# ScalarE writes the feature-128 term of every odd slice into PSUM; TensorE adds three products to it instead of making four

## What is computed

```
X = fft(fft(x, axis=1), axis=2).real          # (2, 3008, 256), seen as 6016 tokens
h = X @ w_in;  g = where(h > 0, h, exp(min(h, 0)) - 1);   y = g @ w_out        # 256 -> 2048 -> 256
h2 = y @ w2_in; g2 = max(h2, 0) + alpha * min(h2, 0);     out = g2 @ w2_out    # 256 -> 2048 -> 256
```

## Time and profile before

| | |
|---|---|
| median of 3 runs | 978.06 us (978.02 to 979.47) |
| the profiled execution | 977.41 us |
| its span in the trace | 975.6 us |
| TensorE busy (its matmuls) | 957.6 us, 98% of the span |
| VectorE busy | 793.1 us, 81% |
| ScalarE busy | 625.1 us, 64% |
| GpSimd busy | 169.9 us, 17% |
| first block, from its first up1 to the second block | 47.41 to 476.15 us |

### The profile page before, as it was taken

One profiled execution on the slowest core, in us unless ns is written; L12 is line 12 of the kernel. 1 busy time (PEld: TensorE's weight loads), 2 busy tenths in 40 slices (PEclk: granted clock), 3 DMA queues, 4 the chain that ended last, 5 costly groups with the idle time before them and its releaser, 6 DMA issues.

```text
span 975.6 us, 12207 instructions
## 1 busy us (share of the span) xinstructions
PE 957.6 (98%) x4450; PEld 798.1 (82%) x4450; DVE 793.1 (81%) x891; ACT 625.1 (64%) x816; POOL 169.9 (17%) x184
## 2 busy tenths in 40 slices
PE   7989999999999999999999999999999999999997
PEld 7868888888888888887888888888888888888886
DVE  6489897887887997889798888878879878887765
ACT  3378887887887787777665555555555555555453
POOL 3478231322321551027000000000000000000000
PEclk9999999999999999999999999999999999999999
DMA  9511120210212346231310110011011011000101
GB/s 245 148 42 36 63 79 1 98 43 29 70 44 98 130 151 243 92 119 44 108 38 1 44 43 1 1 44 44 1 44 43 1 39 44 1 1 1 43 1 44
DMA packets 11704, 57.57 MB, mean 59 GB/s; under 512 B 1706, under 2 KB 2666, under 8 KB 8060
## 3 DMA queue, kind: packets, MB, share of 16 engines
q1 hardware_dynamic: 7628, 30.80, 9.4%
q0 software_dynamic: 4016, 25.99, 7.3%
HBM read 32.75 MB, written 24.01 MB: 58 GB/s over the span
## 4 chain that ended last, share of the span: by engine, by line
PE 58%; DVE 2%; issue 1%; ACT 0%; DVEq 0%; ACTq 0%
PE ACC L604 9%; PE ACC L605 9%; PE ACC L606 9%; PE PQ L556 8%; PE PQ L557 8%; PE PQ L558 8%; PE ACC L574 2%; PE ACC L575 2%; PE ACC L579 2%; DVE Gl L884 1%; DVE G L861 1%; PE PQ L537 0%; PE PQ L538 0%; PE PQ L539 0%; PE PQ L543 0%
## 5 line engine op out<-in xcount | busy, mean ns | idle before, releaser
L574 PE MATMUL ACC<-Gh,W 128*128 128x512 f32 x372 | 144.9, 389 | 2.4 <-DVE Gl L884 2.3
L884 DVE SCALAR_TENSOR_TENSOR Gl<-G,Gh 128x1024 fp32r<-128x1024 f32 (+1 forms) x96 | 122.5, 1276 | 27.1 <-ACT Gh L709 26.3
L575 PE MATMUL ACC<-Gl,W 128*128 128x512 f32 x372 | 143.7, 386 | 0.0
L886 DVE TENSOR_TENSOR Gl<-G,Gh 128x1024 fp32r<-128x1024 f32 (+1 forms) x96 | 115.2, 1200 | 17.7 <-ACT Gh L711 17.3
L604 PE MATMUL ACC<-Gh,W 128*128 128x512 f32 x324 | 124.8, 385 | 2.1 <-DVE Gl L886 2.1
L861 DVE SCALAR_TENSOR_TENSOR G<-H,G 128x1024 f32<-128x1024 f32 (+1 forms) x96 | 125.8, 1311 | 1.0 <-ACT G L730 1.0
L711 ACT ACTIVATE Gh<-G 128x1024 fp32r<-128x1024 f32 (+1 forms) x96 | 100.3, 1045 | 39.9 <-DVE G L876 34.7
L606 PE MATMUL ACC<-Gh,W 128*128 128x512 f32 x324 | 124.5, 384 | 0.0
L605 PE MATMUL ACC<-Gl,W 128*128 128x512 f32 x324 | 124.5, 384 | 0.0
L876 DVE SCALAR_TENSOR_TENSOR G<-H,G 128x1024 f32<-128x1024 f32 (+1 forms) x96 | 115.5, 1204 | 3.3
L579 PE MATMUL ACC<-Gh,W 128*128 128x512 f32 x372 | 113.4, 386 | 0.0
(11 more groups left out here) (112 smaller groups left out, 1801.8 us busy)
## 6 DMA issues: line engine op xcount, KB each, us to landing
w_scratch<-stage POOLq DMA_DIRECT2D x4, 1792.0 KB, 7.2
xr<-in_x SPq DMA_DIRECT2D x16, 384.0 KB, 12.5
raw<-in_w POOLq DMA_DIRECT2D x24, 256.0 KB, 4.4
W3a<-w_scratch POOLq DMA_DIRECT2D x3, 1792.0 KB, 11.0
y_scratch<-y_st SPq DMA_DIRECT2D x5, 1024.0 KB, 3.9
y_in<-y_scratch SPq DMA_DIRECT2D x5, 1024.0 KB, 4.8
out_y<-y_st SPq DMA_DIRECT2D x5, 1024.0 KB, 3.9
w_scratch<-stage POOLq DMA_DIRECT2D x4, 1024.0 KB, 4.9
```

The lines of the kernel that those rows point to most:

```text
L574: mm(o, W2[:, f, 0, sl], Gh[:, j, c:c + w], start=f == 0, stop=False)
L575: mm(o, W2[:, f, 0, sl], Gl[:, j, c:c + w], start=False, stop=False)
L884: stt(Gl[:, j, 0:n], G[:, j, 0:n], bias, f32(Gh[:, j, 0:n]), ALU.add, ALU.subtract).then_inc(lo_ready, 1)
```

## The change

For odd f, ScalarE writes `eb * we` into `PQ[:, 1, 0:512]` before up1 (function `extra`): `eb` is the data row of feature 128 copied to all 128 partitions, `we` one weight per partition, both in full fp32. TensorE's three products then add to it with `start=False`, and L544 is left out. Even f keeps the fourth product. `W1e` holds half the slices. What is new at the start: a third row set (`e_row`) through DRAM and a broadcast load of it in each tile, the weights through DRAM into a column per slice (`load_we`), and a small add on GpSimd. The matmuls of the transforms get other `start` flags, with the same count and sizes.

```
+            def load_we(n, a, b):
+                odd = slice(a // 2, b // 2)
+                sp.wait_ge(w1l_ready, b)
+                sp.dma_start(we_dram[odd, :, :], f32(W1[0:1, a + 1:b:2, 2:4, :])).then_inc(we_stored[n], 16)
+                sp.wait_ge(we_stored[n], 16)
+                sp.dma_start(we_parts[:, odd, :], we_dram[odd, :, :].rearrange("f k p -> p f k"),
+                             allow_slow_non_contiguous=True).then_inc(we_in[n], 16)
+
+            load_we(0, 0, LATE_F)
             load_e(0)
             load_e(1)
+            load_we(1, LATE_F, NF)
...
                 gp.wait_ge(w1e_in, 48 * (n + 1))
+                gp.wait_ge(we_stored[n], 16)
                 gp.memset(f32(W1[0:1, a:b, 2:4, :]), 0.0).then_inc(w1_ready, 1)
+                gp.wait_ge(we_in[n], 16)
+                odd = slice(a // 2, b // 2)
+                gp.tensor_tensor(we[:, odd], we_parts[:, odd, 0], we_parts[:, odd, 1], ALU.add).then_inc(we_ready, 1)
...
-                mm(o, W1[:, f, 0, :], eo(t, 0), start=True, stop=False)
-                mm(o, W1[:, f, 0, :], eo(t, 2), start=False, stop=False)
-                mm(o, W1[:, f, 1, :], eo(t, 0), start=False, stop=False)
-                mm(o, W1e[:, f * PT:(f + 1) * PT], eo(t, 4), start=False, stop=True).then_inc(up_done, 1)
+                if j:
+                    pe.wait_ge(extra_ready, s // 2 + 1)
+                mm(o, W1[:, f, 0, :], eo(t, 0), start=not j, stop=False, skip_group_check=True)
+                mm(o, W1[:, f, 0, :], eo(t, 2), start=False, stop=False, skip_group_check=True)
+                ins = mm(o, W1[:, f, 1, :], eo(t, 0), start=False, stop=j == 1, skip_group_check=True)
+                if not j:
+                    ins = mm(o, W1e[:, f // 2, :], eo(t, 4), start=False, stop=True, skip_group_check=True)
+                ins.then_inc(up_done, 1)
...
+            def extra(s):
+                t, f = s // NF, s % NF
+                if f == 1:
+                    act.wait_ge(eb_in[t % 2], 16 * (t // 2 + 1))
+                if s == 1:
+                    act.wait_ge(we_ready, 1)
+                    act.wait_ge(eol_ready, 1)
+                if s > LATE_F and s - 2 < LATE_F:
+                    act.wait_ge(we_ready, 2)
+                if t < LAST and f == FLIP_AT[t]:
+                    act.wait_ge(eol_ready, t + 2)
+                if s >= 2:
+                    act.wait_ge(comb_ready, s - 1)
+                fn(PQ[:, 1, 0:TW], eb[:, t % 2, :], ACT.Copy, scale=we[:, f // 2:f // 2 + 1]).then_inc(extra_ready, 1)
...
+            extra(1)
             for s in range(S1):
...
                 neg(s)
+                if s % 2 and s + 2 < S1 and not flip_after:
+                    extra(s + 2)
```

More of the change, by code:

```diff
@@ L54, in program @@
     ALU, ACT = mybir.AluOpType, mybir.ActivationFunctionType
-    e_dram = nc.dram_tensor("e_scratch", [2, B * K2, N1], fp32).ap()
+    e_dram = nc.dram_tensor("e_scratch", [3, B * K2, N1], fp32).ap()
+    we_dram = nc.dram_tensor("we_scratch", [NF // 2, 2, PT], fp32).ap()
     y_dram = nc.dram_tensor("y_scratch", [NT, PT, YW], fp32).ap()
@@ L76, in program @@
     W1 = at("W1", o1, [PT, NF, 4, PT], f32r)
-    W1e = at("W1e", o1 + 32 * KB, [PT, F], f32r)
+    W1e = at("W1e", o1 + 32 * KB, [PT, NF // 2, PT], f32r)
+    eb = at("eb", o1 + 36 * KB, [PT, 2, TW], fp32)
     o2 = o1 + 40 * KB
@@ L125, in program @@
     warm = at("warm", o6 + 2048, [PT, 1], fp32)
+    we_parts = at("we_parts", o6 + 2304, [PT, NF // 2, 2], fp32)
+    we = at("we", o6 + 2368, [PT, NF // 2], fp32)
+    e_row = at("e_row", o6 + 2560, [C47 // 2, 2, N1], fp32)
     m64 = [mcf[:, cs * PT:(cs + 1) * PT] for cs in range(2)]
@@ L145, in program @@
         w1e_in, w1_ready, w2_ready = sem("w1e_in"), sem("w1_ready"), sem("w2_ready")
+        we_stored, we_in = [[sem(f"{name}{n}") for n in range(2)] for name in ("we_stored", "we_in")]
+        we_ready, eb_in, extra_ready = sem("we_ready"), [sem("eb_in0"), sem("eb_in1")], sem("extra_ready")
         raw_free, w3_stored, w4_stored, stage_ready = sem("raw_free"), sem("w3_stored"), sem("w4_stored"), sem("stage_ready")
@@ L150, in program @@
         f1_done, t1a_ready, t1b_ready = sem("f1_done"), sem("t1a_ready"), sem("t1b_ready")
-        u_done, uh_ready, ul_ready = sem("u_done"), sem("uh_ready"), sem("ul_ready")
+        u_done, uh_ready, ul_ready, uf_ready = sem("u_done"), sem("uh_ready"), sem("ul_ready"), sem("uf_ready")
         e_zero, e_stored, e_in = sem("e_zero"), sem("e_stored"), [sem("e_in0"), sem("e_in1")]
@@ L249, in _ @@
                 sp.dma_start(e_dram[part, two:two + B, :], f32(e_hl[0:B, part, 1, :])).then_inc(e_stored, 16)
-            sp.wait_ge(e_stored, 64)
+            sp.wait_ge(uf_ready, 2)
+            sp.dma_start(e_dram[2, 0:two, :], e_row[0:two, 0, :]).then_inc(e_stored, 16)
+            sp.dma_start(e_dram[2, two:two + B, :], e_row[0:B, 1, :]).then_inc(e_stored, 16)
+            sp.wait_ge(e_stored, 96)
             sp.wait_ge(e_zero, 1)
@@ L256, in load_e @@
                     sp.dma_start(f32(eo(t, 4)[p:p + 1, :]), src).then_inc(e_in[t % 2], 16)
+                src = e_dram[2, NQ * t:NQ * (t + 1), :].rearrange("q k -> (q k)").partition_broadcast(PT)
+                sp.dma_start(eb[:, t % 2, :], src).then_inc(eb_in[t % 2], 16)
+            def load_we(n, a, b):
[6 more added lines that the diff above has]
+            load_we(0, 0, LATE_F)
             load_e(0)
             load_e(1)
+            load_we(1, LATE_F, NF)
             for t in range(NT - 1):
@@ L322, in _ @@
             ins.then_inc(e_zero, 1)
-            chain(gp.memset(f32(W1e[:, :]), 0.0))
+            chain(gp.memset(f32(W1e[:, :, :]), 0.0))
             for c in range(4):
@@ L340, in move_row @@
                 for p, part in ((0, 2), (32, 3), (64, 2)):
-                    row = f32(W1e[p:p + 1, :]).rearrange("p (f c) -> p f c", f=NF)[:, a:b, :]
-                    gp.dma_start(row, f32(W1[0:1, a:b, part, :])).then_inc(w1e_in, 16)
+                    gp.dma_start(f32(W1e[p:p + 1, a // 2:b // 2, :]), f32(W1[0:1, a:b:2, part, :])).then_inc(w1e_in, 16)
                 gp.wait_ge(w1e_in, 48 * (n + 1))
+                gp.wait_ge(we_stored[n], 16)
                 gp.memset(f32(W1[0:1, a:b, 2:4, :]), 0.0).then_inc(w1_ready, 1)
+                gp.wait_ge(we_in[n], 16)
+                odd = slice(a // 2, b // 2)
+                gp.tensor_tensor(we[:, odd], we_parts[:, odd, 0], we_parts[:, odd, 1], ALU.add).then_inc(we_ready, 1)
             gp.wait_ge(w1l_ready, 2 * (FOLDS - LATE_FOLDS))
@@ L468, in flip1 @@
                         o = PQ[:, c % 2, k * PT:(k + 1) * PT]
-                        ins = mm(o, xr[:, c % XS, k * PT:(k + 1) * PT], m47[:, :], start=True, stop=True)
+                        ins = mm(o, xr[:, c % XS, k * PT:(k + 1) * PT], m47[:, :], start=k % XH == 0, stop=True,
+                                 skip_group_check=True)
                     ins.then_inc(f1_done, 1)
@@ L516, in flip2 @@
                     for n, (c, cs) in enumerate(parts):
-                        ins = mm(o, T1[:, c, :], m64[cs], start=n == 0, stop=n == len(parts) - 1)
+                        ins = mm(o, T1[:, c, :], m64[cs], start=q % (NQ // 2) == 0 and n == 0, stop=n == len(parts) - 1,
+                                 skip_group_check=True)
                 ins.then_inc(f2_done, 1)
@@ L689, in _ @@
                         fn(e_hl[0:r, 0, n, :], ACC[0:r, 0, o:o + N1], ACT.Copy).then_inc(uh_ready, 1)
+                        fn(e_row[0:r, n, :], ACC[0:r, 0, o:o + N1], ACT.Copy).then_inc(uf_ready, 1)
                 t1_copy(c)
@@ L738, in _ @@
                 flip_next = t < LAST and f == FLIP_AT[t] - 1
+                flip_after = t < LAST and f == FLIP_AT[t] - 2
                 if f == 2 and t:
@@ L751, in _ @@
                 if flip_next:
+                    if s % 2 == 0:
+                        extra(s + 1)
                     copy_q(s + 1)
@@ L834, in _ @@
                     dve.wait_ge(uh_ready, 2)
+                    dve.wait_ge(uf_ready, 2)
                     for n, (r, o) in enumerate(U_PARTS):
```

## The result

The changed kernel took 980.90 us (median of 11 runs, 979.37 to 981.80), the kernel before 978.54 beside it (11 runs, 977.17 to 981.10): ratio 1.0023, 95% interval 1.0014 to 1.0032. It is slower by about 2.4 us, where 976.6 was predicted and 0.09 given to "slower". The profiled execution took 981.02 us with a span of 979.2; that of before took 977.41 and 975.6.

What follows compares the result with a forecast made beforehand. TensorE was taken as the bound mid-block, VectorE as the bound or close to it at 60 to 80 and 440 to 460 us. 10.9 - 4.0 - 2.6 - 2.0 - 0.9 = 1.4 us, so 978.06 becomes 976.6; range 973.8 to 979.2.

Steps and rivals of the forecast that it cites:

- The saving of 0.226 a product: Odd slices of the first block: 48 removed TensorE products give back 0.226 us each, 10.9 us if TensorE is the bound.
- The instruction of 0.56: ScalarE's queue: each of 48 added 512-column activations takes 0.56 us, close to the nearest row, a copy from SBUF.
- The joints: Five hand-overs between tiles and four flips at f = 8, where slack is gone: 4.0 and 2.6 us lost.
- 0.79 each: Loss at each of five hand-overs between tiles: 0.56 of delay plus 0.23 of lost saving, 4.0 us in all.
- 0.66 each: Loss at each of four flips at f = 8: up1 0.35 later, 0.23 saving lost, 0.08 after a wait; 2.6 in all.
- The last tile: TensorE waits for g_lo: three odd slices give nothing (0.7), plus 0.2 for a later g_hi; 0.9 us lost.
- Tile 0: Start of the first block, VectorE the bound up to slice 8: 2.0 us of losses together.
- the 0.56 at down1(2): Tile 0, slice 2: g_hi stands behind the extra activation for slice 5, so down1 loses 0.56 us.
- The loads at nothing: Start: the new loads and broadcast cost nothing, with 11 us of cover before the first up1.
- No price for a wait inside a slice: TensorE's new semaphore before the fourth product costs zero; the rival had 0.08 us broken overlap, 979.0 us, chance 0.10.
- the joints absorb it: Rival: hand-overs and flips are not pushed or TensorE makes it up; 8.0 us gained, 970.1 us, chance 0.12.
- The second block as long as before: Profile after: the second block, whose code is the same, keeps its length.

Runs made afterwards that it cites:

- k1: Changed kernel with the extra activation moved at nine joints: behind eo_hi and copy_q at flips, behind exp_neg at hand-overs; 976.38 us, ratio 0.9978.
- k11: Changed kernel with the extra activation behind exp_neg at the hand-overs only, flips unchanged; 978.52 us, ratio 0.9988.
- k6: Changed kernel with eight more matmuls into a spent PSUM bank during TensorE's last wait; 980.55 us, ratio 1.0024.
- k13: Changed kernel with GpSimd's arithmetic in tiles 4 and 5 left out, memsets in its place; 976.07 us, ratio 0.9970.
- k2: Changed kernel without the extra activation: three products on odd slices, rank-one term missing there, loads kept; 974.11 us, ratio 0.9952.
- k15: Kernel before with GpSimd's arithmetic in tiles 4 and 5 left out, memsets in its place; 978.12 us, ratio 1.0000.
- k4: Changed kernel with its loads and GpSimd adds, but no extra activation and seven products on every slice; 978.49 us, ratio 0.9999.
- k3: Changed kernel with the extra activation and all seven products on odd slices; 984.62 us, ratio 1.0061.
- k5: k1 with GpSimd's third group of W4 splits waiting until the hand-over to tile 4; 979.49 us, ratio 1.0011.
- k8: Changed kernel with the extra activation behind exp_neg in every odd slice; 977.83 us, ratio 0.9992.
- k7: k5 with the eight added matmuls of k6 in the last wait; 977.75 us, ratio 0.9988.
- k10: k1 with slice 3 of tile 4 keeping TensorE's fourth product, plus k6's eight matmuls in the last wait; 975.51 us, ratio 0.9974.
- k12: Kernel before with the eight added matmuls of k6 in its last wait; 978.33 us, ratio 0.9988.

## Why the prediction was wrong, by its own steps

The three stages first. Predicted for the first block was a gain of 1.4; the profiled run shows a loss of 1.45, so 2.85 were missed there. Another 1.7 of the profiled run and an open share of the median is the clock at the end. The rest is the start, which is not the change.

*The saving of 0.226 a product* was right: steady pairs of 4.31 and 4.08, and the slack of g_lo's chain held.

*The instruction of 0.56* has a pitch of 0.61. The sum was made from a row without a per-partition factor. This makes some 0.5 us of the 2.85, by nine joints at 0.05. By the prices of the Trainium skill (ScalarE: Activation LUTs, What ACT_TABLE_LOAD costs) its pitch with a pointer operand is 0.61, an estimate, and the trace agrees (0.61).

*The joints.* Place and mechanism were right, and k1 and k11 show it: moving the instruction back by one or two places at nine joints gives 4.5 us. The waits: 1.17, 0.86, 0.86, 1.42 and 0.51 at the hand-overs where 0.79 each was taken, and 0.63, 0.63, 0.63 and 1.17 at the flips where 0.66 was. Those into and in tiles 2 and 3 fit to 0.07. Those of 1.17 and 1.42 at the hand-overs stand where a scalar_tensor_tensor of the chain ran beside GpSimd: k6, with the same code, has 0.86 in place of the 1.42. The 1.17 at the flip of tile 4 is not GpSimd's: it is 1.08 with GpSimd idle (k13). In the kernel before this flip was the only one of f = 8 with a wait (0.36 at 376.98), and the prediction's rows show the flip of tile 1 alone.

*Tile 4* is the first term mis-sized. It was costed like tiles 1 to 3 (1.45 lost against the full saving) and lost 2.7 (73.57 against 70.8), or 2.2 in k6. Its three waits are 1.42 at the hand-over, 0.36 for a g_lo behind it, and 1.17 at the flip. "0.79 each" and "0.66 each" took all joints as alike.

*The last tile* is the second, and the step that failed: "three odd slices give nothing there (0.7), and I add 0.2 for g_hi that comes later". With the hand-over, 0.9 and 0.79 were taken off, and 2.7 were lost (68.22 against 67.35 - 1.8). k2 splits them: without any extra activation the tile takes 67.63, so none of its eight products gives anything (2.1 lost where 0.9 was taken), and the activation adds 0.6 to that, of which the wait at the hand-over (0.51, and 0.21 in k2) is 0.3. So it is for the most part not g_hi that comes late; it is the saving that has no place to go. The earlier trace rows had the warning: VectorE busy for 19.08 of 20.00 us from 440 to 460. Windows over the whole last tile, of the kernel before and of k2:

```profile
408.80:476.15 67.35, 66.53 (x306) 55.75 (x304) 60.02 (x66) 52.08 (x66) 26.30 (x18) 1.00 0.21 71
```

```profile
404.03:471.66 67.63, 65.44 (x297) 54.14 (x296) 61.68 (x66) 52.11 (x66) 25.32 (x18) 1.00 0.20 71
```

VectorE was busy for 60.02 of 67.35 us before, and TensorE waited twice for g_lo (0.40 at 444.15 and 0.75 at 453.18). VectorE's load is not fixed either: the same instruction takes 1.08 or 2.18 us, and the sum took the durations of before as constants. k13 and k15 show what the pair of engines makes of the difference, 2.15 us in the last tile and 1.2 in tile 4; with GpSimd idle the last tile loses the hand-over alone. The kernel before hides most of the long instructions behind TensorE. Why tile 4 of the changed kernel meets more of them than that of before (VectorE's L861 and L920, the same instruction, mean 1271 and 1355 ns there) is a matter of when the two engines meet, which no run here controls.

*Tile 0* lost 1.8 where 2.0 was taken, in other parts than those given, so that the sum was near by luck. The first four odd slices give nothing, as told (0.9), but the 0.56 at down1(2) did not come: slice 8 starts 36.11 us behind the first product, where it was 36.03. From slice 8 on only 0.1 of 0.9 comes, where 0.5 was taken off: there TensorE waits for g_lo, 0.27 at 85.81, 0.30 at 90.36 and 0.20 at 99.03. The flip of tile 0 was to cost nothing and has a wait of 0.35 for the extra activation.

*The loads at nothing* was right: k4 has them and takes 978.49, beside 978.43 of the kernel before. *No price for a wait inside a slice* was right in the steady steps, whose odd slices take 4.08 us. Of the rivals none took place as told. The joints give much of the loss back in another order (k1), but no kernel that computes everything comes near the 970.1 of "the joints absorb it". The other side was given too little: every rival named a single price, and none held that several places without slack can be late together.

*The second block as long as before* was wrong for the profiled run. After the last wait of 2.3 us the clock stood at 0.50 and cost 1.5 to 1.7 us. Of the 13 profiled executions with that wait 6 have the fall (after, k1, k3, k5, k8, k11; second block 496.6 to 496.9 us) and 7 have not (495.0 to 495.3); of the 4 in which the wait is filled (k6, k7, k10, k12) none has. The mean clock was 0.997 or less in 8 of 11 runs of the changed kernel, in 10 of 11 of k5 and of k8, 8 of 10 of k15, 5 of 11 of k1, 1 of 11 of k4, and in 16 of 106 of the kernel before. So the share depends on the kernel, but a mean does not tell where the clock was low, and with the wait filled it is still low in 2 of 11 runs (k12), 3 of 12 (k10), 4 of 12 (k6) and 7 of 12 (k7). What decides it stays open, and no median but that of k7 shows a gain by the filling. What it is worth in a median can be estimated: the 16 low runs of the kernel before took 980.3 us in the mean and its other 90 took 978.5, and in the changed kernel it is 981.1 (8 runs) and 980.3 (3 runs), so 0.8 to 1.8 a run. With 8 of 11 in place of 16 of 106 that is 0.5 to 1.0 us, which would fit the 0.9 that the 1.45 of the first block leave of the 2.4; that is argued, not shown.
